# First value means written by ScalarE, keys sliced in three pieces, the projection one step sooner, waits per bank, spread weights in two buffers

## The chip, the cores and the metric

The kernel runs on one core of a Trainium2 chip. The metric is the device time of one execution in microseconds (us); less is better. The engines of the core are PE (TensorE, matmuls; PEld is its weight load), DVE (VectorE), ACT (ScalarE), POOL (GpSimd) and SP (SyncE, which here only issues DMAs). They run their own queues in order and meet at semaphores.

## The reference, cut to what matters

Three layers follow one another, on 2 batches of 768 rows:

```python
# 1: attention over a window of +-15 rows and 24 block summaries
k_sum = k.reshape(B, H, nb, block, D).max(axis=3)      # block = 32, nb = 24
v_sum = v.reshape(B, H, nb, block, D).mean(axis=3)
scores = concat(masked(scale * q @ k.T), scale * q @ k_sum.T + log(block))
x = softmax(scores) @ concat(v, v_sum)
# 2: four experts, each a causal attention with its own wq, wk, wv, wo; top 2 of 4 by a gate
for e in range(4):
    a = softmax(causal(scale * (x @ wq[e]) @ (x @ wk[e]).T))
    out += weight_of_expert(e) * (a @ (x @ wv[e]) @ wo[e])
# 3: token mixing, then channel mixing
u = out + (relu(out.T @ w_tok1) @ w_tok2).T
return u + relu(u @ w_ch1) @ w_ch2
```

## The kernel before, in words

**Order.** Batch 0 and batch 1 each run attention, projections, expert attention and token mixing (`sequence(b, more)`), then four groups of 384 rows run channel mixing (`group`). Each engine's program is written out by hand, step by step, with the step number k; what an engine does within a step, and so what waits behind what, is the order of the lines in its own `sequence`. Batch 0 is the one trip of a hardware loop (`Fori(0, B - 1)`), batch 1 is written out behind it.

**Attention, steps k = 2 to 15.** A unit u (0 to 11) is 128 query rows (t = u % 6) of four heads (q = u // 6, two pairs of heads). Here S(u), T(u) and V(u) are its scores (`a_scores`), its transposes (`a_transpose`) and its products with the values (`a_values`) on PE. At step k PE does S(k), T(k-2), V(k-3). DVE takes the maxima and normalises (`a_maxima`), ACT takes the exponentials (`a_exps`). ACT and DVE each copy half of the transposes (`a_to_sbuf`, tile PTA) and each write a half of the result in split precision: ACT XT_h (`a_x_hi`), DVE XT_l (`a_x_lo`), both for unit k-4. Semaphore `a_xl` counts the XT_l.

**Keys.** ACT copies windows of the keys KP, scaled, to KW (`key_windows`, L839, three pieces of four windows for each pair r, counted once by `a_kwin`). DVE adds block maxima (`key_maxima`). Pairs 2 and 3 are done at steps 3 and 4.

**Means of the values.** DVE sums blocks of VT (`value_sums`), PE turns the sums (`means`), ACT copies them scaled to VS, and SP sends VS by DMA to rows 96 to 119 of all 12 windows of VW (`place_means`, L329, waits for `a_vs`). For q = 0 this is done before step 2 (`a_first_means`, bank ps_o), for q = 1 at unit 5. V(0) and V(6) wait for the DMA (`ld_vs`). In SP's queue `load_keys(0, 3)`, the second half's queries and values and the weights stand behind `place_means(0, 0)`.

**Projections.** P0 to P7 (`m_project`) are 12 matmuls each: P0, P1, P4, P5 give queries, P2, P3, P6, P7 keys; P4 to P7 are for the second 384 rows and need XT of all 12 units (`a_xl`). Each result goes through ACT (`m_project_hi`, L870, two copies for queries, four for keys) and DVE (`m_project_lo`, L1072, as many). P0 is issued at step 13. Then come value products `m_value(0)` and `m_value(1)`.

**Expert attention, steps k = 0 to 16.** 14 units (`UNITS`), at step k scores(k), transposes(k-2), values(k-3). `m_weights` (DVE) writes the gate weight over the denominator, spread over 64 columns each, to the one buffer `wide`; `m_spread` (PE, then ACT) turns it to SPREAD; `m_normalise` (DVE) multiplies. All DVE work of `m_weights(0)` stands behind the gate's chain.

**Token mixing.** `m_token1`, `m_token2` on PE, `add_tokens` and `sum_x2` on DVE, `store_u` on ACT. The scores of units 0, 1 and 2 of the next batch are issued ahead of its tiles 2, 4 and 6, and behind the first of them `a_first_means(b + 1)`.

## Time and profile before

| | us |
|---|---|
| median of 3 runs | 492.0 (491.32 to 492.31) |
| profiled execution, its own time | 491.06 |
| its span, first to last instruction | 489.3 |
| PE busy | 450.5 (92%) |
| DVE busy | 249.3 (51%) |
| ACT busy | 191.1 (39%) |
| mean granted TensorE clock | 0.979 of full |

Busy times are sums over the whole span, which holds stages with different limits; the change touches those ahead of channel mixing.

### The profile page before, as it was taken

To read this page: it belongs to the slowest core of one execution; us is meant where nothing else is said; L and a number is where in the kernel's file an instruction comes from. 1 tells how busy PE (TensorE), PEld (TensorE's weight loads), DVE (VectorE), ACT (ScalarE), POOL (GpSimd) and SP (SyncE) were. 2 spreads that over 40 slices of the span, in tenths; PEclk is the share of its full clock that TensorE was granted. 3 is DMA by queue.
4 is the path that set the end of the run, shared out by engine and by line. 5 is a ranking of instruction groups with operands and counts; after the bars stand their busy time and mean duration, and the time that the engine had idled before them with its cause. 6 is when DMAs were issued, how large, how long until landed. Compare 5 with 4: busy or idle time off the path is not lost.

```text
span 489.3 us, 8326 instructions
## 1 busy us (share of the span) xinstructions
PE 450.5 (92%) x3254; PEld 382.8 (78%) x3254; DVE 249.3 (51%) x512; ACT 191.1 (39%) x574; POOL 29.1 (6%) x35
## 2 busy tenths in 40 slices
PE   7577989899978789898989999999999999999997
PEld 3355889587755569886868799889988999889985
DVE  4598483877647994848894565311212121212201
ACT  5468463655322885646771244201211021002200
POOL 3032960000000000000000000000000000000000
PEclk9599998999998999999999999999999999999999
DMA  8457371000383036000004550004001300020001
GB/s 281 127 178 176 109 256 68 1 2 0 98 269 110 3 89 261 1 0 1 2 1 129 201 188 1 8 36 150 2 0 44 118 32 0 21 76 32 0 23 43
DMA packets 19555, 38.38 MB, mean 78 GB/s; under 512 B 2112, under 2 KB 6592, under 8 KB 19520
## 3 DMA queue, kind: packets, MB, share of 16 engines
q1 hardware_dynamic: 17792, 34.75, 22.0%
q10 hardware_dynamic: 1728, 3.15, 1.7%
q8 instruction: 24, 0.39, 0.3%
q14 instruction: 11, 0.09, 0.1%
HBM read 30.42 MB, written 6.29 MB: 75 GB/s over the span
## 4 chain that ended last, share of the span: by engine, by line
PE 76%; DVE 14%; DMA 4%; issue 3%; ACT 2%; POOL 0%; ACTq 0%; DVEq 0%; POOLq 0%
PE ps_s L494 37%; PE ps_t L494 22%; PE ps_o L494 6%; PE ps_x L494 5%; DMA VW<-VS 3%; PE ps_t L632 3%; DVE KL L1072 2%; DVE nmaxA L1033 2%; DVE vsum L1180 1%; DVE PTA L1051 1%; DVE nmaxM L1122 1%; DVE ksum L1169 1%; DMA u_rows<-US 1%; ACT KH L870 1%; DVE US L1193 1%
## 5 line engine op out<-in xcount | busy, mean ns | idle before, releaser
L494 PE MATMUL ps_s<-UT_h,ch_h 128*128 128x384 f32 x192 | 65.0, 338 | 0.1
L494 PE MATMUL ps_s<-UT_h,ch_l 128*128 128x384 f32 x192 | 64.9, 338 | 0.0
L494 PE MATMUL ps_s<-UT_l,ch_h 128*128 128x384 f32 x192 | 64.9, 338 | 0.0
L1314 DVE SCALAR_TENSOR_TENSOR HID_l<-ps_s,HID_h 128x384 fp32r<-128x384 f32 x48 | 26.7, 557 | 66.0 <-ACT HID_h L1012 66.0
L1012 ACT ACTIVATE HID_h<-ps_s 128x384 fp32r<-128x384 f32 x48 | 23.6, 491 | 93.8 <-PE ps_s L494 93.7
L494 PE MATMUL ps_t<-ch_h,HID_h 128*128 128x512 f32 x144 | 56.7, 394 | 0.0
L494 PE MATMUL ps_t<-ch_h,HID_l 128*128 128x512 f32 x144 | 56.2, 390 | 0.0
L494 PE MATMUL ps_t<-ch_l,HID_h 128*128 128x512 f32 x144 | 56.1, 389 | 0.0
L1322 DVE TENSOR_TENSOR OS<-ps_t,UR 128x512 f32<-128x512 f32 x12 | 8.3, 691 | 83.6 <-PE ps_t L494 83.6
L829 ACT ACTIVATE PA<-ps_s,nmaxA 128x120 f32<-128x120 f32 x96 | 33.4, 375 | 19.4 <-DVE nmaxA L1033 19.4
L494 PEld LDWEIGHTS ps_s<-UT_h,ch_h 128*128 128x128 f32 x192 | 36.0, 188 | 0.6 <-DVE UT_l L1198 0.5
L494 PEld LDWEIGHTS ps_s<-UT_l,ch_h 128*128 128x128 f32 x192 | 36.1, 188 | 0.1
L885 ACT ACTIVATE PM<-ps_s,nmaxM 128x128 f32<-128x128 f32 (+5 forms) x48 | 30.1, 633 | 15.5 <-DVE nmaxM L1122 15.4
L494 PEld LDWEIGHTS ps_s<-UT_h,ch_l 128*128 128x128 f32 x192 | 36.0, 188 | 0.0
L1122 DVE TENSOR_REDUCE nmaxM<-ps_s 128x1 f32<-128x640 f32 (+5 forms) x28 | 26.7, 952 | 13.4 <-PE ps_s L494 13.4
L494 PEld LDWEIGHTS ps_t<-ch_h,HID_l 128*128 128x128 f32 x144 | 27.0, 188 | 5.8
L494 PEld LDWEIGHTS ps_t<-ch_l,HID_h 128*128 128x128 f32 x144 | 27.1, 188 | 5.3
L494 PEld LDWEIGHTS ps_t<-ch_h,HID_h 128*128 128x128 f32 x144 | 27.0, 188 | 5.3
L632 PE MATMUL ps_t<-ident,PM 128*128 128x128 f32 x168 | 23.3, 275 | 2.9 <-DVE PTM L1136 2.9
L547 PE MATMUL ps_t<-ident,PA 128*120 128x128 f32 x96 | 16.6, 300 | 9.2 <-DVE PTA L1051 3.8
L926 ACT ACTIVATE UT_h<-ps_o 128x512 fp32r<-128x512 f32 x8 | 4.8, 598 | 51.7 <-PE ps_o L711 47.8
L494 PE MATMUL ps_s<-KH,QS 128*128 128x512 f32 (+3 forms) x64 | 23.7, 376 | 0.0
(165 smaller groups left out, 909.7 us busy)
## 6 DMA issues: line engine op xcount, KB each, us to landing
VW<-in_vw SPq DMA_DIRECT2D x12, 384.0 KB, 8.2
KP<-in_kT SPq DMA_DIRECT2D x8, 384.0 KB, 6.8
QT<-in_qT SPq DMA_DIRECT2D x12, 256.0 KB, 5.3
VT<-in_vT SPq DMA_DIRECT2D x8, 384.0 KB, 6.8
u_rows<-US ACTq DMA_DIRECT2D x12, 256.0 KB, 2.1
ch_raw<-in_ch SPq DMA_DIRECT2D x4, 768.0 KB, 6.6
US<-u_rows SPq DMA_DIRECT2D x4, 768.0 KB, 5.8
ch_raw<-in_ch SPq DMA_DIRECT2D x12, 256.0 KB, 4.8
```

Source lines behind the costliest of these rows:

```text
L494: return pe.matmul(out, lhsT, rhs, start=start, stop=stop)
L547: last = pe.transpose(ps_t[0:KC, j // 2, (j % 2) * P:(j % 2 + 1) * P], PA[:, u % 3, j, :], ident[:, :])
L632: last = pe.transpose(ps_t[:, at_ // 512, at_ % 512:at_ % 512 + P], PM[:, u % 3, at_:at_ + P], ident[:, :])
L829: last = act.activation(PA[:, u % 3, j, :], ps_s[u % 2][:, j % 2, (j // 2) * KC:(j // 2 + 1) * KC], ACT.Exp, bias=nmaxA[:, u % 4, j:j + 1] ...
L870: last = act.activation((KH if key else QS)[own[(i + to) % 2], 2 * pair + i, n * GS:(n + 1) * GS], bank[g % 4][own[i], 0:GS], ACT.Copy, sc ...
L885: last = act.activation(PM[:, u % 3, part], ps_s[u % 2][:, :, :].rearrange("p a c -> p (a c)")[:, part], ACT.Exp, bias=nmaxM[:, t, e:e + 1 ...
L1012: act.activation(HID_h[:, m, :], bank[m % 4][:, 0:GS], ACT.Relu).then_inc(g_hh, 1)
L1033: dve.tensor_reduce(nmaxA[:, u % 4, :].rearrange("p (j r) -> p r j", r=2), ps_s[u % 2][:, :, 0:2 * KC].rearrange("p r (j c) -> p r j c", j=2),
L1072: last = dve.scalar_tensor_tensor(out, bank[g % 4][own[i], 0:GS], 1.0 if key else SCALE, hi, ALU.mult, ALU.subtract)
L1122: dve.tensor_reduce(nmaxM[:, t, experts[0]:experts[0] + n], ps_s[u % 2][:, :, :].rearrange("p a c -> p (a c)")[:, 0:n * stride] .rearrange ...
L1314: dve.scalar_tensor_tensor(HID_l[:, m, :], bank[m % 4][:, 0:GS], 0.0, HID_h[:, m, :].bitcast(F32), ALU.max, ALU.subtract).then_inc(g_hl, 1)
L1322: dve.tensor_tensor(OS[:, j, :], bank[4 + j % 2], UR[:, j, :], ALU.add).then_inc(g_o, 1)
```

## The change

What it does, by parts:

- **Start.** 16 warming matmuls in place of 20. The first query load holds 3 tiles of 128 rows, not 2. Values are loaded ahead of the rest of the queries. DVE sums the values of pair 0 and 1 between the maxima, in two parts.
- **First means.** `a_first_means` is issued at step 3, behind T(1), to bank ps_x. ACT writes the means itself to the first 4 windows (q = 0) or 2 windows (q = 1) of VW and then to VS; the DMA takes the other windows. V(0) and V(6) wait for ACT (`a_vd`), V(2t) from the first window on that the DMA writes waits for `ld_vs`; V(1) waits for `a_vs`.
- **Keys.** `key_windows` takes one piece of both pairs at a time, at steps 3, 4 and 5; scores wait for the piece that they read.
- **Projection.** P0 at step 12, P1 at 13, P2 at 14, P3 at 15. Waits for P0 and P2 are for their own bank and weights. Scores 0 and 1 of the experts wait for the bank that they overwrite, not for the last projection.
- **Spread weights.** `wide` has two buffers and lies in the weights' staging tile. The first spread and its normalisation are a step later, at 4.
- **Order at step 15.** The first `m_token1` goes ahead of transposes(13).
- **Loop.** Both batches are written out.

```diff
-N_WARM = 20
+N_WARM = 16
+CUT_AT = (3, 4, 5)
-Q_FIRST = 2 * P
+Q_FIRST = 3 * P
+DIRECT = (4, 2)
-SPREAD_AT = [LAST[_t] + 3 for _t in range(TQ)]
+SPREAD_AT = [LAST[_t] + (4 if _t == 0 else 3) for _t in range(TQ)]
...
+        wide = raw[:, :, 0:E * HD]
...
                 sp.wait_ge(a_vs, 2 * b + q + 1)
-                sp.dma_start(VW[WK:KC, q, :, :], VS[WK:KC, q, :].unsqueeze(1).broadcast_to([NB, NW, 4 * D])
-                             ).then_inc(ld_vs[q], 16)
+                sp.dma_start(VW[WK:KC, q, DIRECT[q]:NW, :],
+                             VS[WK:KC, q, :].unsqueeze(1).broadcast_to([NB, NW - DIRECT[q], 4 * D])).then_inc(ld_vs[q], 16)
...
             for r in range(2):
+                load_values(0, r)
+            for r in range(2):
                 load_queries(0, r)
-            for r in range(2):
-                load_values(0, r)
...
-            sp.wait_ge(a_kwin, B * PAIRS)
+            sp.wait_ge(a_kwin, B * PAIRS * 3)
...
-                    pe.wait_ge(a_kwin, b * PAIRS + 2 * q + 2)
                     pe.wait_ge(ld_qf[q], b * 16 + 16)
+                if t % 2 == 0:
+                    pe.wait_ge(a_kwin, b * PAIRS * 3 + 6 * q + t + 2)
...
-                means(ps_o, b, 0).then_inc(a_vm, 1)
+                means(ps_x, b, 0).then_inc(a_vm, 1)
...
                 if t == 0:
+                    pe.wait_ge(a_vd, 2 * b + q + 1)
+                if t == DIRECT[q] // 2:
                     pe.wait_ge(ld_vs[q], b * 16 + 16)
+                if u == 1:
                     pe.wait_ge(a_vs, 2 * b + 1)
...
+                if g % 2 == 0 and g < 4:
+                    pe.wait_ge(c_lo, g // 2 + 1)
+                    pe.wait_ge(a_exp, b * NU + NU - 1 + g // 2)
                 if g == 0:
                     pe.wait_ge(a_xl, b * NU + (NU - TQ // 2))
                 if g == 4:
...
-                if u == 0:
-                    pe.wait_ge(m_pl, b * 8 + 8)
+                if u < 2:
+                    pe.wait_ge(m_pl, b * 8 + 6 + 2 * u)
...
+                    if k == 3:
+                        a_first_means(b)
                     if 3 <= k <= NU + 2:
                         a_values(b, k - 3)
-                    if k == NU + 1:
-                        pe.wait_ge(c_lo, N_QK)
-                    if k > NU:
-                        m_project(b, k - NU - 1)
-
-                for g in range(3, 8):
+                    if k >= NU:
+                        m_project(b, k - NU)
+
+                for g in range(4, 8):
                     m_project(b, g)
...
+                    if k == SPREAD_AT[0]:
+                        m_spread(b, 0)
+                    if k == MU + 1:
+                        for m in range(KT):
+                            m_token1(b, 0, m)
                     if 2 <= k <= MU + 1:
                         m_transpose(b, k - 2)
                     if k - 1 in TURN_AT:
                         m_out_project(b, TURN_AT.index(k - 1))
-                    if k == MU + 1:
-                        for m in range(KT):
-                            m_token1(b, 0, m)
-                    if k in SPREAD_AT:
-                        m_spread(b, SPREAD_AT.index(k))
+                    if k in SPREAD_AT[1:]:
+                        m_spread(b, 1 + SPREAD_AT[1:].index(k))
...
                         a_scores(b + 1, SCORES_BEFORE.index(t))
-                        if t == SCORES_BEFORE[0]:
-                            a_first_means(b + 1)
...
-            with pe.Fori(0, B - 1) as b:
-                sequence(b, True)
-            sequence(B - 1, False)
+            for b in range(B):
+                sequence(b, b < B - 1)
...
+            def key_windows(b, q, i):
+
+                for r in (2 * q, 2 * q + 1):
+                    if i == 0:
+                        act.wait_ge(ld_k[r], b * 16 + 16)
+                    act.activation(KW[:, r, 4 * i:4 * i + 4, 0:WK], windows(r, 4 * i), ACT.Copy, scale=SCALE).then_inc(a_kwin, 1)
+
+            def a_means(b, q, sums):
+
+                n = DIRECT[q]
+                act.activation(VW[WK:KC, q, 0:n, :], sums.unsqueeze(1).broadcast_to([NB, n, 2 * P]), ACT.Copy,
+                               scale=1.0 / BLOCK).then_inc(a_vd, 1)
+                act.activation(VS[WK:KC, q, :], sums, ACT.Copy, scale=1.0 / BLOCK).then_inc(a_vs, 1)
...
                     if k <= NU + 1:
                         a_to_sbuf(b, k - 2)
+                    if k == 3:
+                        a_first_means(b)
                     if 3 <= k < NU:
                         a_exps(b, k)
-                    if k in KEYS_AT:
-                        key_windows(b, (2 + KEYS_AT.index(k),))
-                    if k > NU:
-                        m_project_hi(b, k - NU - 1)
+                    if k in CUT_AT:
+                        key_windows(b, 1, CUT_AT.index(k))
+                    if k >= NU:
+                        m_project_hi(b, k - NU)
...
-                if t >= 1:
-                    dve.wait_ge(m_d, b * TQ + t)
-                dve.tensor_tensor(wide[:, :].rearrange("p (e d) -> p e d", e=E),
+                if t == 0:
+                    dve.wait_ge(c_lo, N_TOK2)
+                if b * TQ + t >= 2:
+                    dve.wait_ge(m_d, b * TQ + t - 1)
+                dve.tensor_tensor(wide[:, t % 2, :].rearrange("p (e d) -> p e d", e=E),
...
-                    if k > NU:
-                        m_project_lo(b, k - NU - 1)
+                    if k >= NU:
+                        m_project_lo(b, k - NU)
...
+                    if k == SPREAD_AT[0]:
+                        m_normalise(b, 0)
...
-            a_maxima(0, 1, 0)
-            value_sums(0, (0, 1))
-            a_maxima(0, 2, 1)
+            a_maxima(0, 1)
+            value_sums(0, (0,))
+            a_maxima(0, None, 0)
+            a_maxima(0, 2)
+            value_sums(0, (1,))
+            a_maxima(0, None, 1)
```

## Rows read from the trace of the kernel before

**Rows 1.** Busy time in channel mixing: stretch, its length, PE, PEld, DVE, ACT, POOL, clock, DMA.

```profile
282.00:489.00 207.00, 203.95 (x1044) 186.09 (x1044) 51.75 (x87) 35.94 (x71) 0.00 (x0) 1.00 0.12 45
```

**Rows 2.** What PE waited for, 188 to 224 us: total, times, longest.

```profile
PE ps_x L647 <- DVE wide L1146: 1.7, 1, 1.7
PE ps_s L494 <- DVE KL L1072: 1.7, 1, 1.7
```

**Rows 3.** Busy times as in group 1: three stretches of equal length behind gaps of PE.

```profile
74.40:77.80 3.40, 3.40 (x18) 3.40 (x17) 0.69 (x1) 1.56 (x9) 0.00 (x0) 0.50 0.32 122
146.10:149.50 3.40, 3.40 (x9) 2.66 (x9) 1.29 (x2) 0.00 (x0) 0.00 (x0) 0.51 0.36 75
208.80:212.20 3.40, 3.40 (x31) 3.36 (x31) 0.69 (x1) 1.83 (x10) 0.00 (x0) 1.00 0.00 0
```

**Rows 4.** Timeline, attention of batch 0: start, us, instruction, idle before.

```profile
17.65 0.50 SPq L310 DMA_DIRECT2D KP<-in_kT  x1
21.83 1.15 PE L494 MATMUL ps_o<-PTA,VW 120*64 120x64 f32 x16 [3.07 <-DMA VW<-VS]
27.98 0.65 DVE L1033 TENSOR_REDUCE nmaxA<-ps_s 128x4 f32<-128x480 f32 x1
30.20 0.94 DVE L1180 TENSOR_REDUCE vsum<-VT 128x24 f32<-128x768 f32 x1
42.67 0.66 DVE L1033 TENSOR_REDUCE nmaxA<-ps_s 128x4 f32<-128x480 f32 x1 [0.94 <-PE ps_s L494]
```

**Rows 5.** DMA issues of 17.6 and of 21.5 us: KB, us to landing.

```profile
KP<-in_kT SPq DMA_DIRECT2D x1, 384.0 KB, 5.5
VT<-in_vT SPq DMA_DIRECT2D x2, 384.0 KB, 7.6
```

**Rows 6.** Groups of ACT by shape: count, busy us, mean ns, idle before.

```profile
L916 ACT ACTIVATE X_h<-ps_x 128x512 fp32r<-128x512 f32 x12 | 7.2, 596 | 9.8 <-PE ps_x L494 9.7
L850 ACT ACTIVATE VS<-ps_t 24x256 f32<-24x256 f32 x2 | 0.8, 377 | 3.5 <-PE ps_t L494 3.5
```

**Rows 7.** Timeline, token mixing of batch 0 and attention of batch 1.

```profile
145.04 0.62 PE L494 MATMUL ps_o<-ident,vsum 128*24 128x128 f32 x4 [2.50 <-DVE vsum L1180]
156.03 0.65 DVE L1033 TENSOR_REDUCE nmaxA<-ps_s 128x4 f32<-128x480 f32 x1
159.16 0.73 PE L494 MATMUL ps_o<-PTA,VW 120*64 120x64 f32 x16
178.13 0.66 DVE L1033 TENSOR_REDUCE nmaxA<-ps_s 128x4 f32<-128x480 f32 x1 [0.67 <-PE ps_s L494]
```

**Rows 8.** Timeline, batch 0: XT_l of unit 8, P0, P2, its copies, P4.

```profile
49.57 0.41 DVE L1058 TENSOR_TENSOR XT_l<-ps_o,XT_h 128x256 fp32r<-128x256 f32 x1
50.97 0.44 PE L494 MATMUL ps_s<-XT_h,wq_h 128*128 128x384 f32 x1
56.14 0.34 PE L494 MATMUL ps_s<-XT_h,wk_h 128*128 128x384 f32 x1
58.45 4.09 ACT L870 ACTIVATE KH<-ps_s 64x384 fp32r<-64x384 f32 x8 [0.72 <-PE ps_s L494]
60.47 4.56 DVE L1072 SCALAR_TENSOR_TENSOR KL<-ps_s,KH 64x384 fp32r<-64x384 f32 x8 [1.53 <-ACT KH L870]
60.36 0.34 PE L494 MATMUL ps_s<-XT_h,wq_h 128*128 128x384 f32 x1
```

**Rows 9.** Timeline, experts of batch 0: copy of transposes(1), then transposes(2).

```profile
90.44 0.68 DVE L1136 COPY PTM<-ps_t 128x512 f32<-128x512 f32 x1
91.22 0.85 PE L632 MATMUL ps_t<-ident,PM 128*128 128x128 f32 x6
```

**Rows 10.** Timeline, end of the experts of batch 0: transposes(13), their copy, the values.

```profile
125.82 0.87 PE L632 MATMUL ps_t<-ident,PM 128*128 128x128 f32 x6
126.73 0.69 DVE L1136 COPY PTM<-ps_t 128x512 f32<-128x512 f32 x1 [0.20 <-PE ps_t L632]
128.22 1.53 PE L494 MATMUL ps_o<-PTM,VE 128*64 128x128 f32 x24
```

More of the change, by code:

```diff
@@ L139, in program @@
         gate_rank = sb("gate_rank", [P, TQ, E], F32)
-        wide, end_wide = at("wide", [P, E * HD], F32, gate_at)
-        assert end_wide <= place[0]
         gate_w = sb("gate_w", [P, TQ, E], F32)
@@ L253, in program @@
         a_vsum = sem("a_vsum")
-        a_vm = sem("a_vm"); a_vs = sem("a_vs")
+        a_vm = sem("a_vm"); a_vs = sem("a_vs"); a_vd = sem("a_vd")
         a_s = sem("a_s")
@@ L646, in m_spread @@
                 for r in range(EP):
-                    last = pe.transpose(ps_x[:, r * P:(r + 1) * P], wide[:, r * P:(r + 1) * P], ident[:, :])
+                    last = pe.transpose(ps_x[:, r * P:(r + 1) * P], wide[:, t % 2, r * P:(r + 1) * P], ident[:, :])
                 last.then_inc(m_d, 1)
@@ L832, in a_exps @@
                 last.then_inc(a_exp, 1)
-            def key_windows(b, pairs):
-                for r in pairs:
-                    act.wait_ge(ld_k[r], b * 16 + 16)
-                    for w in range(0, NW, 4):
-                        last = act.activation(KW[:, r, w:w + 4, 0:WK], windows(r, w), ACT.Copy, scale=SCALE)
-                    last.then_inc(a_kwin, 1)
+            def key_windows(b, q, i):
[8 more added lines that the diff above has]
+                act.activation(VS[WK:KC, q, :], sums, ACT.Copy, scale=1.0 / BLOCK).then_inc(a_vs, 1)
             def a_first_means(b):
                 act.wait_ge(a_vm, b + 1)
-                act.activation(VS[WK:KC, 0, :], ps_o[WK:KC, 0:2 * P], ACT.Copy, scale=1.0 / BLOCK).then_inc(a_vs, 1)
+                a_means(b, 0, ps_x[WK:KC, 0:2 * P])
             def a_to_sbuf(b, u):
@@ L849, in a_to_sbuf @@
                 if u == MEANS_AT:
-                    act.activation(VS[WK:KC, 1, :], ps_t[WK:KC, 1, 2 * P:4 * P], ACT.Copy, scale=1.0 / BLOCK).then_inc(a_vs, 1)
+                    a_means(b, 1, ps_t[WK:KC, 1, 2 * P:4 * P])
                 if u >= 2:
@@ L978, in sequence @@
                 if more:
-                    key_windows(b + 1, (0, 1))
+                    for i in range(3):
+                        key_windows(b + 1, 0, i)
                 m_out_hi(b, TQ - 1)
@@ L998, in _ @@
             act.activation(sumA[:, 0, 0:1], denA[:, 0, 0:1], ACT.Exp)
-            key_windows(0, (0, 1))
+            for i in range(3):
+                key_windows(0, 0, i)
             for k in range(3):
                 a_exps(0, k)
-            a_first_means(0)
-            with act.Fori(0, B - 1) as b:
-                sequence(b, True)
-            sequence(B - 1, False)
+            for b in range(B):
+                sequence(b, b < B - 1)
             def group(g, more, first=False):
@@ L1223, in sequence @@
                         value_sums(b, (2 + SUMS_AT.index(k),))
-                    if k > NU:
-                        m_project_lo(b, k - NU - 1)
-                for g in range(3, 8):
+                    if k >= NU:
+                        m_project_lo(b, k - NU)
+                for g in range(4, 8):
                     m_project_lo(b, g)
@@ L1301, in _ @@
             a_maxima(0, 0)
-            a_maxima(0, 1, 0)
-            value_sums(0, (0, 1))
-            a_maxima(0, 2, 1)
-            with dve.Fori(0, B - 1) as b:
-                sequence(b, True)
-            sequence(B - 1, False)
+            a_maxima(0, 1)
[4 more added lines that the diff above has]
+            a_maxima(0, None, 1)
+            for b in range(B):
+                sequence(b, b < B - 1)
             def group(g, more, first=False):
```

20 lines of the change are left out of this document (9 added, 11 removed).

## The prediction

> **What bounds the kernel now.** I read the view by stage first. Channel mixing, from 282 us on, keeps PE busy 203.95 of 207 us at full clock [rows 1]; the change touches none of it. So the question is the 282 us ahead of it, and there the waits of PE and what ends them. In the timeline of attention (two stretches of some 30 us) DVE is the engine without a pause: maxima, normalising, copies and XT_l of one unit follow the last one's, and key maxima and value sums come on top. A gain of PE or ACT there counts only where DVE itself stood idle: 0.94 us behind V(6) in batch 0 and 0.67 in batch 1 [rows 4, 7], and at the start, where V(0) waited 3.07 us for the DMA of the means [rows 4]. In projections and experts PE sets the pace, with two waits in each batch, 1.7 us each: for the last KL ahead of the first scores, and for `wide` [rows 2]. In token mixing PE waited 2.50 us for value sums [rows 7].
>
> The sum is made against the profiled execution, 491.06 us (span 489.3). The median is 492.0.
>
> **The start and attention of batch 0: -1.2 us (from -4 to +1).** Fewer warming matmuls, values sooner and the new order of DVE bring V(0) ahead. Laid out with the durations of the trace, T(1) ends near 15.5 us, the means' matmuls near 16.4, ACT's direct write near 17.7, and V(0) starts there instead of at 21.83 [rows 4]: 4.1 us. But ACT's `a_vs` comes only then, near 18.0. SP's queue stands on it, and behind it `load_keys(0, 3)`, which was issued at 17.65 [rows 4] and landed 5.5 us later [rows 5]; now it is issued near 18.8 and lands near 24. At step 3 ACT now takes the first piece of both pairs, so it waits for that landing, with XT_h, PTA and all exponentials behind it. DVE comes to the maxima of unit 5 near 26.2 instead of 27.98 [rows 4], and next stands at the sums of VT, which are behind in the same SP queue: they were issued at about 21.6 and took 7.6 us [rows 5], and DVE used them at 30.20 [rows 4] with little to spare. The broadcast is a third smaller, which gives the queue back about what the later issue costs, so they land near 29.4. Left at unit 6: 0.7 us. At unit 5's means ACT writes two windows more, 512 elements a row: the row of that length takes 0.60 [rows 6], some 0.5 when instructions overlap. V(6) no longer waits, 0.94 of DVE's idle time [rows 4]. 0.7 - 0.5 + 0.94 makes 1.2. The upper end of the gain is V(0)'s whole 4.1, the lower a landing 2 us later than I put it.
>
> **Attention of batch 1: +1.4 (0 to +2.5).** Here the means were long ready; now they stand between T(1) and V(0). The matmuls take 0.6 [rows 7]. For ACT's write of 1,024 elements the trace has no row. From 256 elements in 0.38 to 512 in 0.60 [rows 6] it grows by 0.22 per 256, which gives 1.04; the bounds are 0.60 and twice that. So V(0) comes 1.7 us after its old place (159.16 less what came before) [rows 7], S(4) stands behind it, and DVE waits for S(4): 1.6 us less the little it had to spare. ACT's second direct write adds 0.45; the 0.67 of idle time behind V(6) goes [rows 7]. The keys in three pieces take the same 12 copies on ACT; the wait they save on PE lay beside a busy DVE, so nothing is counted.
>
> **Projections: +1.7 in each batch, +3.4 (-1.2 to +2.5 each).** P0 at step 12 needs XT_l of unit 8, which DVE ends at 49.98 [rows 8]; P0 began at 50.97. But T(11) and V(10) were already done then. P0, P1 and V(11) took 5.17 (50.97 to 56.14) and a product 2.11 (56.14 to 60.36 is two) [rows 8], so a V with its changes of shape is 0.95, and T is as long as the means' 0.6 [rows 7]. P0 at 50.05 + 2.11 + 0.6 + 0.95 + 2.11 + 0.95 puts P2 at 56.8, 0.6 us later than now. The large item is P4. It waits for XT_l of unit 11. That stands at step 15 of DVE's queue, and step 14 now holds the copies of P2, a key product: ACT starts its four copies 2.3 us after P2's first matmul (56.14 to 58.45) and takes 4.09/8 x 4 = 2.05, DVE then 4.56/8 x 4 = 2.28 and XT_l 0.41 [rows 8]. That is 7.1 us after P2's start; P3 ends 4.2 us after it (56.14 to 60.36) [rows 8]. PE stands 2.85 us ahead of P4, where it had no wait. Before, only the cheap copies of P1 stood there. Against this the first scores no longer wait for the last KL, 1.7 [rows 2]: they need the copies of P5, done two products sooner. 0.6 + 2.85 - 1.7 makes 1.7.
>
> **Spread weights: -0.1 each, -0.2 (0 to -1.5 each).** The wait of 1.7 for `wide` [rows 2] goes from its place, but DVE worked without pause through that stretch. Its copy of transposes(1) ends at 91.12, and transposes(2), which need it, began at 91.22 [rows 9]. PE now waits there.
>
> **Order at step 15: +0.65 each, +1.3 (0 to +1.4).** Before, `m_token1` (six matmuls, 1.4 us of the 2.40 between transposes(13) at 125.82 and the values at 128.22) covered their copy, 126.73 to 127.42 [rows 10]. Now the transposes begin 1.4 us later, their copy ends near 128.8, and the values at 128.9. The cover is gone, nothing is won.
>
> **Token mixing of batch 0: -4.3 (-2.7 to -4.8).** PE loses the wait of 2.50 and the 0.6 of matmuls [rows 7], and with them the low stretch that followed, 3.4 us at half the clock [rows 3], worth up to 1.7: 4.8 at most. DVE still does the sums there, so it sets what follows: added up through its queue, the maxima of unit 2 begin near 152.0 instead of 156.03 [rows 7]. The end of the loop, where PE waited for nothing that the trace shows, gives 0.3.
>
> **The clock: +2.0 (-1.4 to +2.0).** The granted clock has two levels here, 2.4 and 1.2 GHz. Behind the 1.7 us wait for KL it fell in batch 0 and not in batch 1 [rows 3]: in the same 3.4 us PE began 18 matmuls in the one and 31 in the other, so the fall cost 13/31 of 3.4, 1.4 us. It also fell behind the wait of 2.50. The stall ahead of P4, 2.85 us, is longer than both gaps, and what follows it is bound by PE. I take a fall in each batch, 3.4/2 = 1.7 of dense projections, less the 1.4 of before. The Trainium skill ("TensorE: Matmul & The Clock Gate", Part 1: The HAM clock gate) says that half the clock is the default and activity lifts it, and that a kernel with repeated idle gaps pays for the warming each time; by it the two new stalls cost this, and batch 1 of before was luck.
>
> **The sum.** -1.2 + 1.4 + 3.4 - 0.2 + 1.3 - 4.3 + 2.0 = +2.4 us, 493.5 us. The median stood 0.9 above the profiled execution; since the changed kernel is taken with both falls already, I add nothing for that.
>
> **Rivals.** *The clock holds in one batch or both.* The sum less 1.7 or 3.4: 491.8 or 490.1. For it: batch 1 held after 1.7 us [rows 3]. Against it: the longer gap. *The start keeps its gain* (the one on the faster side): ACT at step 3 finds pair 3's keys landed within about 3 us of their issue, and VT as early; then V(0)'s 4.1 reaches the units behind and the time is 493.5 - 2.9 = 490.6. It decides from a landing near 22 us. Against it stand the 5.5 and 7.6 us [rows 5]. *The new waits for DMA come last.* In batch 1 SP sends the windows from 4 on only after ACT's write, near 157. Batch 0's whole broadcast, issued just ahead of 17.65, held V(0) until 21.83 [rows 4]; at 4 to 5 us they land as V(2) wants them. With 1 us there and batch 0's VT a further 2 late, +3: 496.5. *The change does as it says and P4 is not held*: only if ACT and DVE drained P2's copies within P3, and 4.3 us of copies do not fit in 2.1; I give it no chance of its own.
>
> **Chances.** The forecast 0.42; clock kept in one batch 0.19, in both 0.11; start keeps its gain 0.15; DMA last 0.13. No change that this kernel's measurement can tell is within 0.2%, 1.0 us about 492.0. Faster takes the two cases at 490.1 and 490.6, slower the forecast but a small part and the last, same the case at 491.8 and that part. Range 489.9 to 496.0: from the case with the clock kept to just short of the DMA case. The forecast's own range is 492.4 to 495.0.
>
> **What would show it.** PE idle for 2 to 3 us ahead of P4 in both batches, ended by DVE's XT_l, with a low clock behind it; no wait for KL ahead of the first scores; PE waiting for DVE's PTM copy where it waited for `wide`; V(0) in batch 0 near 17.7 but exponentials of unit 4 only near 25, behind a wait of ACT for KP; V(0) of batch 1 behind ACT's write. It is wrong if P4 follows P3 without a gap, if ACT's write takes far from 1 us, or if KP and VT land sooner than now.

## The result, and the profile after

The changed kernel took 499.7 us (median of 4 runs, 497.37 to 501.9) against 491.7 (4 runs) of the kernel before on the same chip: ratio 1.0165, 95% interval 1.0107 to 1.0223. A second set of runs gave 499.35 us, ratio 1.015 (1.0127 to 1.0172). It is 8 us slower; I had forecast 2.4 in the sum and 1.5 against the median, in a range that ended at 496. The direction was right and the size was not.

The rows below are of the second profiled execution (499.63 us, span 497.8), which lies nearer to the median than the first (501.9 us). Channel mixing is what it was [rows 1]; stretch, length, PE, PEld, DVE, ACT, POOL, clock, DMA:

```profile
290.80:497.80 207.00, 203.80 (x1044) 185.94 (x1044) 51.51 (x86) 35.94 (x71) 0.00 (x0) 1.00 0.13 45
```

To see where the 8 us arise I took seven instructions of DVE that close a stage and set their starts side by side. The timeline of before (two more of them stand in [rows 8] and [rows 7]: XT_l of unit 8 at 49.57, maxima of unit 2 of batch 1 at 156.03):

```profile
80.65 1.22 DVE L1122 TENSOR_REDUCE nmaxM<-ps_s 128x4 f32<-128x1024 f32 x1 [4.92 <-PE ps_s L494]
132.69 0.68 DVE L1187 TENSOR_TENSOR US<-X_h,X_l 128x512 f32<-128x512 f32 x1
183.98 0.41 DVE L1058 TENSOR_TENSOR XT_l<-ps_o,XT_h 128x256 fp32r<-128x256 f32 x1
213.52 1.23 DVE L1122 TENSOR_REDUCE nmaxM<-ps_s 128x4 f32<-128x1024 f32 x1 [3.62 <-PE ps_s L494]
274.54 0.68 DVE L1198 TENSOR_TENSOR UT_l<-ps_o,UT_h 128x512 fp32r<-128x512 f32 x1
```

The same seven of the changed kernel:

```profile
46.99 0.41 DVE L1072 TENSOR_TENSOR XT_l<-ps_o,XT_h 128x256 fp32r<-128x256 f32 x1
79.60 1.22 DVE L1136 TENSOR_REDUCE nmaxM<-ps_s 128x4 f32<-128x1024 f32 x1 [3.08 <-PE ps_s L495]
134.44 0.68 DVE L1203 TENSOR_TENSOR US<-X_h,X_l 128x512 f32<-128x512 f32 x1
155.92 0.65 DVE L1047 TENSOR_REDUCE nmaxA<-ps_s 128x4 f32<-128x480 f32 x1
187.30 0.41 DVE L1072 TENSOR_TENSOR XT_l<-ps_o,XT_h 128x256 fp32r<-128x256 f32 x1
219.80 1.22 DVE L1136 TENSOR_REDUCE nmaxM<-ps_s 128x4 f32<-128x1024 f32 x1 [3.08 <-PE ps_s L495]
283.50 0.68 DVE L1214 TENSOR_TENSOR UT_l<-ps_o,UT_h 128x512 fp32r<-128x512 f32 x1
```

The differences of neighbouring starts, against the terms of my sum (the clock's +2.0 put where I had put it):

| stage, up to | before | after | change | forecast |
|---|---|---|---|---|
| start and attention 0, XT_l of unit 8 | 49.57 | 46.99 | -2.6 | -1.2 |
| projections 0, maxima of scores(1) | 31.08 | 32.61 | +1.5 | +2.0 |
| experts 0, first US | 52.04 | 54.84 | +2.8 | +0.55 |
| token mixing 0, maxima of unit 2 | 23.34 | 21.48 | -1.9 | -4.3 |
| attention 1, XT_l of unit 8 | 27.95 | 31.38 | +3.4 | +1.4 |
| projections 1, maxima of scores(1) | 29.54 | 32.50 | +3.0 | +3.4 |
| experts and token mixing 1 | 61.02 | 63.70 | +2.7 | +0.55 |
| sum | | | +9.0 | +2.4 |

**The wait ahead of P4 is there, the one for KL is gone.** What PE waited for from 193 to 231 us, the counterpart of [rows 2] (total, times, longest):

```profile
PE ps_s L495 <- DVE XT_l L1072: 2.7, 1, 2.7
PE ps_t L640 <- ACT PM L897: 1.8, 1, 1.8
PE ps_t L640 <- DVE PTM L1150: 0.4, 1, 0.4
```

**The clock fell in more places than I had counted.** Busy times as above: at P0 of batch 0, in attention of batch 1, in the experts of batch 0 and 1, and behind the wait ahead of P4 of batch 1:

```profile
47.60:51.00 3.40, 3.40 (x11) 3.40 (x12) 0.00 (x0) 0.00 (x0) 2.95 (x3) 0.52 0.42 151
156.00:166.20 10.20, 8.47 (x83) 5.80 (x84) 5.71 (x15) 6.70 (x27) 0.00 (x0) 0.53 0.17 47
92.00:95.40 3.40, 3.40 (x20) 2.22 (x17) 0.89 (x3) 1.46 (x5) 0.00 (x0) 0.52 0.00 0
231.20:234.60 3.40, 2.96 (x21) 2.10 (x18) 1.77 (x5) 2.92 (x8) 0.00 (x0) 0.59 0.00 0
201.42:204.82 3.40, 3.40 (x11) 3.40 (x12) 2.07 (x4) 0.00 (x0) 0.00 (x0) 0.55 0.00 0
62.60:66.00 3.40, 3.40 (x19) 3.40 (x20) 2.05 (x4) 0.97 (x2) 3.05 (x3) 1.00 1.01 282
```

The last row is P4 of batch 0: behind the same wait of 2.70 us the clock held there. In the first profiled execution of this kernel the same place was at half speed:

```profile
63.80:67.20 3.40, 3.35 (x10) 3.35 (x11) 2.12 (x4) 0.00 (x0) 2.14 (x2) 0.50 0.94 306
```

So the same program with the same wait pays for the fall in one execution and not in another, 10 matmuls started in 3.4 us against 19.

What a fall in the experts costs can be read too. In the run with the end of token mixing filled (below), whose experts have the same instructions, the clock held in both batches:

```profile
81.13:134.41 53.28, 48.62 (x400) 38.53 (x399) 38.17 (x81) 28.76 (x77) 0.00 (x0) 1.00 0.04 11
218.30:280.51 62.21, 57.25 (x441) 45.89 (x441) 46.14 (x93) 33.77 (x85) 0.00 (x0) 1.00 0.15 52
```

That is 53.28 us against 54.84 of the table in batch 0, and 62.21 against 63.70 in batch 1: 1.56 and 1.49 us.

**The start.** Timeline of batch 0, counterpart of [rows 4]:

```profile
15.88 1.02 ACT L850 ACTIVATE VW<-ps_x 24x1024 f32<-24x1024 f32 x1 [0.16 <-PE ps_x L495]
17.04 1.15 PE L495 MATMUL ps_o<-PTA,VW 120*64 120x64 f32 x16 [1.20 <-ACT VW L850]
18.24 1.40 SPq L311 DMA_DIRECT2D KP<-in_kT  x1
23.74 0.52 ACT L845 ACTIVATE KW<-KP 128x384 f32<-128x384 f32 x1 [4.66 <-DMA KP<-in_kT]
26.11 0.65 DVE L1047 TENSOR_REDUCE nmaxA<-ps_s 128x4 f32<-128x480 f32 x1
28.32 0.94 DVE L1196 TENSOR_REDUCE vsum<-VT 128x24 f32<-128x768 f32 x1
```

V(0) comes at 17.04, ACT waits 4.66 us for the keys and the maxima of unit 5 begin at 26.11; I had said 17.7, a wait, and 26.2. Only the values were sooner than I put them: the sum of VT began at 28.32 without a wait, 1.9 us ahead of its old place [rows 4], where I had left 0.7. The gain of the start differs between executions: the six traces with the same instructions up to there put XT_l of unit 8 from 45.72 to 48.36, which is 1.2 to 3.9 us ahead of before. And it does not need ACT's direct write: the run of start, key pieces and bank-wise wait (below), which places the means by DMA alone, has XT_l of unit 8 at 46.99 as well.

**Token mixing.** Timeline and, last, one DMA issue (KB, us to landing):

```profile
149.33 0.69 DVE L1203 TENSOR_TENSOR US<-X_h,X_l 128x512 f32<-128x512 f32 x1 [1.99 <-DMA u_rows<-US]
160.60 1.02 ACT L850 ACTIVATE VW<-ps_x 24x1024 f32<-24x1024 f32 x1 [0.60 <-PE ps_x L495]
161.76 1.14 PE L495 MATMUL ps_o<-PTA,VW 120*64 120x64 f32 x16 [1.20 <-ACT VW L850]
u_rows<-US ACTq DMA_DIRECT2D x1, 256.0 KB, 5.6
```

PE no longer waits for the value sums, but DVE now stands 1.99 us at its next sum, since that writes a buffer of US whose store landed only 5.6 us after its issue, while the loads of batch 1 shared the DMA engines. That takes back what PE gained. Most of the 1.9 us of the table is not the missing wait but the clock. The run with the projection part alone (below) keeps token mixing as it was before, with the same wait of 2.50, but there the clock held. Token mixing of before, and of that run:

```profile
132.69:156.03 23.34, 19.32 (x119) 14.04 (x118) 14.56 (x27) 5.12 (x20) 0.00 (x0) 0.93 0.70 216
142.44:164.23 21.79, 17.76 (x118) 12.87 (x118) 14.56 (x26) 5.13 (x20) 0.00 (x0) 1.00 0.82 232
```

So 1.55 of the 23.34 us were the low clock behind the wait, and against 21.79 the changed kernel's 21.48, also at full clock, is 0.3 us. Writing the loop out gave nothing: the run of the bank-wise wait alone, with the loop written out, took 23.37 there.

**Order at step 15.** The values of the last unit wait for the copy, as forecast (+0.7 us):

```profile
129.21 0.69 DVE L1150 COPY PTM<-ps_t 128x512 f32<-128x512 f32 x1 [1.64 <-PE ps_t L640]
129.96 1.53 PE L495 MATMUL ps_o<-PTM,VE 128*64 128x128 f32 x24 [0.56 <-DVE PTM L1150]
```

### The profile page after: what moved, and what is told of

Same layout as the page of the kernel before. It is cut to its first block, busy times and chain, and to the rows that moved or that the text cites. A ratio compares the mean times of both kernels' runs of the same rounds, so it can differ in the third digit from the quotient of the medians.

```text
span 500.1 us, 8325 instructions
## 1 busy us (share of the span) xinstructions
PE 457.7 (92%) x3250; PEld 388.4 (78%) x3250; DVE 250.5 (50%) x512; ACT 193.1 (39%) x578; POOL 28.5 (6%) x35
## 4 chain that ended last, share of the span: by engine, by line
PE 74%; DVE 15%; issue 5%; ACT 3%; DMA 2%; SPq 0%; ACTq 0%; POOL 0%; DVEq 0%; POOLq 0%
PE ps_s L495 36%; PE ps_t L495 21%; PE ps_o L495 7%; PE ps_x L495 6%; PE ps_t L640 2%; DVE nmaxA L1047 2%; DVE PTA L1065 1%; DVE nmaxM L1136 1%; DVE XT_l L1072 1%; DMA u_rows<-US 1%; DVE vsum L1196 1%; DMA KP<-in_kT 1%; DVE US L1209 1%; DVE KL L1086 1%; ACT KH L882 1%
## 5 line engine op out<-in xcount | busy, mean ns | idle before, releaser
L1136 DVE TENSOR_REDUCE nmaxM<-ps_s 128x1 f32<-128x640 f32 (+5 forms) x28 | 26.7, 953 | 10.6 <-PE ps_s L495 10.5
L495 PE MATMUL ps_o<-PTM,VE 128*64 128x128 f32 x336 | 24.5, 292 | 2.0 <-DVE PTM L1150 1.1
L549 PEld LDWEIGHTS ps_t<-ident,PA 128*120 128x120 f32 x96 | 11.3, 150 | 19.1 <-DVE PA L1057 10.9
```

The lines of the kernel that those rows point to most:

```text
L495: return pe.matmul(out, lhsT, rhs, start=start, stop=stop)
L549: last = pe.transpose(ps_t[0:KC, j // 2, (j % 2) * P:(j % 2 + 1) * P], PA[:, u % 3, j, :], ident[:, :])
L1136: dve.tensor_reduce(nmaxM[:, t, experts[0]:experts[0] + n], ps_s[u % 2][:, :, :].rearrange("p a c -> p (a c)")[:, 0:n * stride] .rearrange ...
```

## The experiments

Ratios are to the kernel before on the same chip, with 95% intervals. Where a stretch is given for batch 1, it is from the start of XT_l of unit 8 to that of the maxima of scores(1), as in the table: 29.54 before, 32.50 changed.

### Parts taken out of the changed kernel

**The changed kernel again.** No edit.

> The changed kernel as it is, to narrow its interval and to be the base of the three runs beside it. Both theories: ratio to before about 1.016 (499 to 500 us).

Measured: 499.35 us (497.88 to 500.04), 1.015 (1.0127 to 1.0172). It is the base of what follows.

**Without the projection part**, on PE, ACT and DVE alike, with P0 to P3 and their waits as before:

```diff
-                    if k >= NU:
-                        m_project(b, k - NU)
+                    if k > NU:
+                        m_project(b, k - NU - 1)
```

> The changed kernel with the projections back at their old steps (k > NU, no waits on the single splits). Theory A, the recorded sum: the part costs 1.7 us in each batch, so 3.4 us less than the changed kernel, and 2 to 3 us more if the low-clock stretches that follow P0 and P4 (46.7 to 53.5, 63.8 to 67.2 and 203.7 to 207.1 us in the trace of after) go too: 492 to 496 us. Theory B, the loss is in the spread step and the low clock that follows it: at most 1 us less than the changed kernel, 498 to 500 us.

Measured: 487.15 us, 0.9925 (0.9897 to 0.9953): 12.2 us less than the changed kernel, and faster than before. This part alone carries more than the whole loss; theory B fell, and the gain is larger than theory A had (492 to 496). Of it my sum held 0.6 and 2.85 in each batch and 2.0 for the clock, 8.9. By the traces (spans 497.8 and 485.1), 8.2 us less are in the projections of the two batches; most of the rest is in stretches that the edit does not touch, 1.6 in the experts of batch 0 and 1.4 in attention of batch 1, where the clock held, or was low for less time, in this trace. The stretch of batch 1 is 27.72:

```profile
179.88 0.41 DVE L1071 TENSOR_TENSOR XT_l<-ps_o,XT_h 128x256 fp32r<-128x256 f32 x1
207.60 1.22 DVE L1135 TENSOR_REDUCE nmaxM<-ps_s 128x4 f32<-128x1024 f32 x1 [3.08 <-PE ps_s L495]
```

**Without the spread part**: one buffer `wide` again, and

```diff
-SPREAD_AT = [LAST[_t] + (4 if _t == 0 else 3) for _t in range(TQ)]
+SPREAD_AT = [LAST[_t] + 3 for _t in range(TQ)]
...
-                    if k in SPREAD_AT[1:]:
-                        m_normalise(b, 1 + SPREAD_AT[1:].index(k))
+                    if k - 3 in LAST:
+                        m_normalise(b, LAST.index(k - 3))
```

> The changed kernel with the spread of query tile 0 back at step 3, the single buffer of the spread weights and the normalisation in its old place. Theory A, the recorded sum: the part gives 0.1 us in each batch, so the time stays within 0.5 us of the changed kernel. Theory B, from the trace of after, in which the stretch from the row maxima of scores(3) to out_project(0) grew by 1.9 us in batch 0 and 2.0 us in batch 1, with a wait of 1.83 us for the exponentials and a low clock from 94.5 to 97.9 us: about 4 us less than the changed kernel, 495 to 496 us.

Measured: 497.6 us (495.04 to 502.42), 1.012 (1.0075 to 1.0165). The interval overlaps that of the changed kernel: no more than a hint of 2 us, less than theory B wanted.

**Without the means part**: no direct writes, and

```diff
-                    if k == 3:
-                        a_first_means(b)
...
+                        if t == SCORES_BEFORE[0]:
+                            a_first_means(b + 1)
```

> The changed kernel with the first means back ahead of step 2 (before the loop, and in the token mixing of batch 0) and all means placed by DMA alone. Theory A, the recorded sum: the sum of values comes back into token mixing (4.3 us) and attention of batch 1 gets 1.4 us back: about 3 us more than the changed kernel. Theory B, from the trace of after: token mixing gained only 2.0 us and attention of batch 1 lost 2.5 us, so within 1 us of the changed kernel.

Measured: 499.55 us, 1.0167 (1.0136 to 1.0199). No difference, against my recorded 3 us. In its trace token mixing is back at 24.6 us and attention of batch 1 at 27.7: what the part gains in the one (3.2 us) it loses in the other (3.7). Much of both is the clock, which was low in this trace's token mixing from 146 to 153 us.

### The projection part by itself

**The projection part alone** on the kernel before (the loop over batches written out, as in the change).

> The kernel before with the projections one step sooner and their waits, and the batch loop written out; nothing else. Theory A (the part costs by itself: transposes and values of the last units fall between the projections, 0.6 us, and P4 waits 2.85 us for XT_l of unit 11, in each batch; the wait of 1.7 us for KL ahead of the first scores stays): about +7 us, and +1.5 us more for each stretch of low clock behind that wait: 499 to 502 us. Theory B (the cost comes only together with the earlier start and the other parts, as the trace without the part hints, since it is 12 us faster than the changed kernel): +3 us or less, at most 495 us.

Measured: 501.4 us (496.46 to 502.84), 1.0186 (1.0136 to 1.0237). Theory A. The part needs no help from the others. In batch 1 the stretch is 32.92, with the clock up throughout; PE there waited 2.71 us for XT_l ahead of P4, and 1.7 us for KL as before.

**XT of unit 11 ahead of the copies of projection 2**, in the changed kernel, on ACT and in the same way on DVE:

```diff
-                    if k >= NU:
+                    if k >= NU and k != NU + 2:
+                        if k == NU + 3:
+                            m_project_hi(b, 2)
                         m_project_hi(b, k - NU)
```

> The changed kernel, but ScalarE and VectorE make XT_h and XT_l of unit 11 ahead of their copies of projection 2. Theory A: XT_l of unit 11 is then ready 2 us before P4, the wait of 2.7 us in each batch is gone, and with it the low clock in P4 to P7 (1.5 us each): 8 us less than the changed kernel, 490.5 to 492 us. Theory C (the four copies of a key projection are themselves late, and P5 or P6 waits for a bank instead): 2 us less at most, 497 us.

Measured: 493.18 us (488.61 to 494.97, 11 runs), 1.0032 (1.0 to 1.0064): 6.2 us less than the changed kernel. The stall is the queue position of XT_l, as the prediction had it; the time lies between the theories, nearer to A. It is still 6 us above the kernel without the part. Most of that goes with the clock: three of the eleven executions took 488.6 to 489.9 us at a mean clock of 0.975 to 0.979, eight took 492.1 to 495.0 at 0.965 to 0.969.

**The wait ahead of P4 filled**: 12 matmuls on constants.

```diff
                 if g == 4:
+                    for _ in range(12):
+                        mm(ps_t[:, 0, :], ident_b[:, :], ident_b[:, :].unsqueeze(1).broadcast_to([P, 4, P]), True, True)
                     pe.wait_ge(a_xl, b * NU + NU)
```

> The changed kernel with 12 matmuls on constants (128x512 bf16, written to a bank that nobody reads) between P3 and the wait for XT_l of unit 11. Theory A, the low clock in P4 to P7 follows from the idle 2.7 us of TensorE: P4 and P5 take 4.4 us instead of 5.9 us in both batches and the time falls by about 3 us, to 496 us. Theory D, the falls come whatever TensorE does there: P4 and P5 take 5.9 us as before and the time is that of the changed kernel or up to 0.5 us more (499.4 to 500 us).

Measured: 497.56 us, 1.0137 (1.0102 to 1.0172), 1.8 us less. The interval overlaps that of the changed kernel, and theory A wanted 3 us with both batches at the low clock; so the cause is read from the trace. The stretch of batch 1 and the clock behind the fillers:

```profile
188.39 0.42 DVE L1075 TENSOR_TENSOR XT_l<-ps_o,XT_h 128x256 fp32r<-128x256 f32 x1
219.49 1.23 DVE L1139 TENSOR_REDUCE nmaxM<-ps_s 128x4 f32<-128x1024 f32 x1 [3.07 <-PE ps_s L496]
202.50:205.90 3.40, 3.40 (x19) 3.40 (x20) 2.07 (x4) 0.97 (x2) 0.00 (x0) 1.00 0.00 0
```

31.10 us: the wait is as long as it was, the clock is up, and 1.40 us are gone. So the price of this part in batch 1 comes apart. Without it 27.72; with XT_l in time (the run with both places mended, below) 28.13, so 0.41 for T(11) and V(10) among the projections; the stall 2.97; the clock 1.40.

**Without projection and spread parts.**

> The changed kernel without the projection part and without the spread part. Theory A, the recorded sum (spread -0.1 us in each batch): the same as without the projection part alone, 487.2 us. Theory B, from the traces: the stretch from the row maxima of scores(3) to those of scores(8) is 16.65 us without the spread part and 17.16 us with it where the clock stays up, 18.7 us where it falls: 0.5 to 2 us less in each batch, 483 to 486 us.

Measured: 488.67 us (486.23 to 493.08, 12 runs), 0.995 (0.9914 to 0.9986). No gain over 487.15, so not theory B; the intervals of the two runs overlap, and theory A's 487.2 is not excluded.

### What the other parts are worth

**The bank-wise wait alone** on the kernel before:

```diff
-                if u == 0:
-                    pe.wait_ge(m_pl, b * 8 + 8)
+                if u < 2:
+                    pe.wait_ge(m_pl, b * 8 + 6 + 2 * u)
```

> The kernel before with the first scores waiting bank by bank for the projections, and the batch loop written out; nothing else. Theory A, the recorded sum: the wait of 1.7 us for KL ahead of the first scores goes in each batch: 3.4 us less than before, 488 us. Theory E (the first scores start 1.7 us sooner, but the next ones wait for the last KL instead, and the clock falls as before): 1 us less at most, 490.5 us or more.

Measured: 489.87 us, 0.994 (0.9905 to 0.9976): 2.3 us less, between the theories. In the trace its 1.8 us are all there, 27.72 against 29.54:

```profile
183.16 0.41 DVE L1056 TENSOR_TENSOR XT_l<-ps_o,XT_h 128x256 fp32r<-128x256 f32 x1
210.88 1.22 DVE L1120 TENSOR_REDUCE nmaxM<-ps_s 128x4 f32<-128x1024 f32 x1 [3.08 <-PE ps_s L494]
```

**Start, key pieces and bank-wise wait**, the good half below. On the kernel before:

```diff
-N_WARM = 20
+N_WARM = 16
-Q_FIRST = 2 * P
+Q_FIRST = 3 * P
...
-                    if k in KEYS_AT:
-                        key_windows(b, (2 + KEYS_AT.index(k),))
+                    if k in CUT_AT:
+                        key_windows(b, 1, CUT_AT.index(k))
```

with the order of loads and of DVE's first maxima and sums as changed.

> The kernel before with the start (16 warming matmuls, three query tiles first, values ahead of the other queries, one sum of values between the maxima), the keys in three pieces, the bank-wise wait and the loop written out; without the projection, means, spread and order parts. Theory A, from the traces: 3.4 us by the bank-wise wait, 1 to 3 us by the start, and none of the 1.3 us of the order and of the 1 to 4 us of the spread: 484 to 486 us. Theory E: the start's gain is lost again behind the placing of the means by DMA, which is late as before: 488 us.

Measured: 485.74 us (484.8 to 487.88), 0.9875 (0.9828 to 0.9923). Theory A: these three are the good half of the change.

**Without projection part and order**: as the run without the projection part, and `m_token1(b, 0, m)` back in its old place at step 15.

```diff
-                    if k == MU + 1:
-                        for m in range(KT):
-                            m_token1(b, 0, m)
...
+                    if k == MU + 1:
+                        for m in range(KT):
+                            m_token1(b, 0, m)
                     if k in SPREAD_AT[1:]:
                         m_spread(b, 1 + SPREAD_AT[1:].index(k))
```

> The changed kernel without the projection part and with the first token product behind the spread again at step 15. Theory A, the recorded sum (order +0.65 us in each batch): 1.3 us less than without the projection part alone: 485.9 us. Theory F (the wait for the copy of the transposed scores only moves): 487.2 us, no difference.

Measured: 488.38 us, 0.9921 (0.9885 to 0.9956). Theory F's 487.2 lies in the interval, theory A's 485.9 does not. The 0.7 us of the order are in its trace (15.6 us from the maxima of scores(12) to the first US, 16.3 with the order), but not in the median.

**Without projection part and means.**

> The changed kernel without the projection part and with all means placed ahead of step 2 and by DMA alone. Theory A, the recorded sum (means -4.3 us in token mixing, +1.4 us in attention of batch 1): 3 us more than without the projection part alone, 490 us. Theory B, from the traces with and without the means part (token mixing 2.3 us shorter with it, attention of batch 1 2.3 us longer at the same clock, 3.7 us longer with the stretches of low clock): 0 to 1.5 us less, 485.6 to 487.2 us.

Measured: 488.73 us, 0.9931 (0.9898 to 0.9965). Between the theories, and not to be told from 487.15.

**The spread part on the good half.**

> The kernel of start, key pieces and bank-wise wait with the spread part. Theory A, the recorded sum: -0.1 us in each batch, 485.5 us. Theory B: 0.5 us more in each batch by the wait for the exponentials of scores(3) ahead of the transposes, and up to 1.5 us more in each by a fall of the clock behind it: 486.7 to 489.7 us.

Measured: 488.53 us (484.53 to 492.72, 12 runs), 0.9925 (0.989 to 0.996). Theory B in direction, though the intervals overlap (0.989 to 0.9923). In the traces batch 1's experts and token mixing take 61.51 us against 61.02, 0.5 more; batch 0's token mixing took 1.3 more, with a low clock from 139 to 149 us. This is where the 0.5 us come from. Timeline without the part (maxima of scores(3), normalisation of tile 0, values of tile 1):

```profile
216.68 0.95 DVE L1123 TENSOR_REDUCE nmaxM<-ps_s 128x2 f32<-128x768 f32 x1
218.89 0.41 DVE L1154 TENSOR_TENSOR OX<-ps_o,SPREAD 128x256 f32<-128x256 f32 x1
220.07 1.09 PE L495 MATMUL ps_o<-PTM,VE 128*64 128x128 f32 x16
```

With it:

```profile
217.57 0.95 DVE L1125 TENSOR_REDUCE nmaxM<-ps_s 128x2 f32<-128x768 f32 x1
219.19 0.68 DVE L1139 COPY PTM<-ps_t 128x512 f32<-128x512 f32 x1
219.97 0.84 PE L632 MATMUL ps_t<-ident,PM 128*128 128x128 f32 x6 [1.82 <-ACT PM L885]
220.92 0.41 DVE L1158 TENSOR_TENSOR OX<-ps_o,SPREAD 128x256 f32<-128x256 f32 x1
221.47 1.09 PE L493 MATMUL ps_o<-PTM,VE 128*64 128x128 f32 x16 [0.44 <-ACT PTM L897]
```

The transposes(2) begin 2.40 us behind the maxima with and without the part (219.08 without), at the end of DVE's copy of transposes(1), 219.87: so far the recorded sum, and the view's "ACT PM" is only the work that ended last by the profile. But the normalisation of tile 0 has moved from 2.21 us behind the maxima to 3.35, behind DVE's maxima of scores(4), and the values of tile 1 write the bank that it reads. They begin at 221.47, 3.90 us behind the maxima, instead of 3.39: 0.5 us. The view names ACT's copy of PTM there, which ended at 221.34, as the normalisation did at 221.33; but that is the copy of transposes(2), and by the program these values read transposes(1) and wait for the normalisation.

### The clock, and a better version

**The end of token mixing filled** in the changed kernel: 10 matmuls on constants ahead of the wait for the last sum.

```diff
                 if more:
+                    for _ in range(10):
+                        mm(ps_o[:, :], ident_b[:, :], ident_b[:, :].unsqueeze(1).broadcast_to([P, 4, P]), True, True)
                     pe.wait_ge(m_u, b * TQ + TQ)
```

> The changed kernel with 10 matmuls on constants ahead of the wait of 2.7 us for the last sum at the end of the token mixing of batch 0; nothing else. Theory A, the low clock of 156 to 167 us follows from this wait: it goes, and attention of batch 1 takes 28 us from the row maxima of unit 2 to XT_l of unit 8 instead of 31.4 us: 3 us less, 496 us. Theory D: it comes all the same, since the wait for the means and the short matmuls of attention are enough: 499 us.

Measured: 496.8 us, 1.0103 (1.0054 to 1.0152), 2.6 us less, with an interval that overlaps that of the changed kernel. It is theory A, though not its 28 us. The low stretch is gone, and attention of batch 1 takes 29.43 us instead of 31.38:

```profile
156.00:166.20 10.20, 7.60 (x122) 5.40 (x122) 7.70 (x18) 8.31 (x35) 0.00 (x0) 1.00 0.17 47
156.21 0.65 DVE L1049 TENSOR_REDUCE nmaxA<-ps_s 128x4 f32<-128x480 f32 x1
185.64 0.41 DVE L1074 TENSOR_TENSOR XT_l<-ps_o,XT_h 128x256 fp32r<-128x256 f32 x1
```

What stays, 29.43 less 27.95, is 1.5 us: my term of 1.4 for the means between T(1) and V(0).

**The good half with its long waits filled**: 6 and 8 such matmuls ahead of the value sums, 10 ahead of the placed means of batch 0, 5 at the end of token mixing. The first of the four places:

```diff
+                for _ in range(8 if b else 6):
+                    mm(ps_o[:, :], ident_b[:, :], ident_b[:, :].unsqueeze(1).broadcast_to([P, 4, P]), True, True)
                 pe.wait_ge(a_vsum, b * PAIRS + 2 * q + 2)
```

> The kernel of start, key pieces and bank-wise wait (485.7 us), with matmuls on constants (128x512 bf16, to a bank in no use) ahead of four waits: 6 and 8 ahead of the sums of values, 10 ahead of the placed means of batch 0, 5 at the end of the token mixing of batch 0. Theory A, the clock falls where TensorE has idled: the low stretches at 14 to 17, 20 to 24 and 143 to 146 us go, 3 us less: 483 us. Theory D, the falls come anyway, and the fillers reach past the waits: 0 to 1 us more, 486 to 487 us.

Measured: 483.87 us, 0.9819 (0.9772 to 0.9867), 1.9 us less than 485.74. The two intervals overlap, though the slowest of these six executions (484.33) is faster than the fastest of those (484.8).

**All waits of attention filled too**, 3 each for units 2 to 11:

```diff
+                    for _ in range(3):
+                        mm(ps_t[:, 0, :], ident_b[:, :], ident_b[:, :].unsqueeze(1).broadcast_to([P, 4, P]), True, True)
                 pe.wait_ge(a_norm, b * NU + (u + 1))
```

> As the run beside it, and 3 such matmuls ahead of the wait for the normalised scores of each of the units 2 to 11 in both batches. Theory A: the low stretch at 48 to 51 us goes too, 1.5 us less than the run beside it, if the fillers (0.64 us at full clock) hide in the waits of 0.7 to 1.5 us. Theory D: where the wait is shorter than 0.64 us the fillers delay the unit, up to 20 times 0.3 us: 3 to 6 us more than the run beside it.

Measured: 486.65 us, 0.9886 (0.9839 to 0.9932). Theory D: the clock is higher (0.993 against 0.989), but fillers that outlast their wait delay the work behind them: attention of batch 1 took 29.18 us, and 27.71 in the run before it, at full clock in both.

**Both places mended in the changed kernel** (XT of unit 11 first, end of token mixing filled).

> The changed kernel with XT_h and XT_l of unit 11 made ahead of the copies of projection 2, and with 10 matmuls on constants ahead of the wait at the end of the token mixing of batch 0. Theory A, the two mends add up (6.2 us and 2.6 us measured singly): 490.5 us, 1 to 2 us less than the kernel before. Theory G, the clock falls in another place once it is kept up here: 493 us, no gain over the first mend alone.

Measured: 488.85 us (487.7 to 492.9, 12 runs), 0.9948 (0.9912 to 0.9985). That is 10.5 us less than the changed kernel, and 0.5% faster than before. The two mends add up, as theory A had it; that they give more than 6.2 and 2.6 lies within the intervals. What the rest of the change costs, in the experts and in attention of batch 1, is less than its start and bank-wise wait give. In this trace the clock fell in attention of batch 1 all the same, some 4 us behind the filled wait (0.64 from 155.0 to 158.4), and attention took 30.50 us. The stretch of batch 1, 28.13:

```profile
181.69 0.42 DVE L1076 TENSOR_TENSOR XT_l<-ps_o,XT_h 128x256 fp32r<-128x256 f32 x1
209.82 1.22 DVE L1140 TENSOR_REDUCE nmaxM<-ps_s 128x4 f32<-128x1024 f32 x1 [3.08 <-PE ps_s L495]
```

**The good half, fillers ahead of `wide` as well** (7 in each batch, and 5 ahead of the waits for the normalised scores of units 9 to 11 of batch 0).

```diff
+                    for _ in range(7):
+                        mm(ps_x[:, :], ident_b[:, :], ident_b[:, :].unsqueeze(1).broadcast_to([P, 4, P]), True, True)
                 pe.wait_ge(m_den, b * (3 * TQ) + (3 * t + 3))
```

> The version with its long waits filled (483.9 us), and 7 such matmuls more ahead of the wait of 1.7 us for the wide weights in each batch and 5 ahead of the waits for the scores of units 9 to 11 of batch 0. Theory A: the low stretches at 44 to 51 and 85 to 88 us go, 482 us. Theory D: fillers (1.5 us and 1.1 us) that reach past their wait take it back: 484 us.

Measured: 482.12 us (480.94 to 482.59), 0.9786 (0.9743 to 0.983): the fastest of all, 2.1% under the kernel before, with an interval from 1.7 to 2.6%. Its page has no slice with a low clock (40 equal slices, tenths):

```profile
PEclk9999999999999999999999999999999999999999
```

## Why the prediction was right in direction and wrong in size

The direction was right by its mechanism: without the projection part the change is faster than before. The size was a miss of 6.6 us in the traces, +9.0 against +2.4.

- **The start, -1.2: measured -2.6** in this trace, and -1.2 to -3.9 over six. Each step up to unit 5 was right to 0.7 us. Mis-sized: the landing of VT, which I took to be at about 29.4; it was there by 28.3.
- **Projections, 0.6 + 2.85 - 1.7: measured in batch 1 +0.41 + 2.97 - 1.82.** The mechanism and its terms hold. What decided was the order of two copies in a queue, and moving them alone (6.2 us) shows it.
- **Spread weights, -0.1 each: measured +0.5.** I costed the buffer and left out the normalisation that moved with it. The values of tile 1 wait for it; this step of the part was not followed.
- **Order, +0.65 each: measured +0.7.** Right in the traces; too small for the medians.
- **Token mixing, -4.3: measured -1.9.** This step failed. Of the 1.9, 1.55 are the low clock that went, for which I had up to 1.7; of the other 2.6 us, 0.3 came. I followed DVE's queue with work alone and left out that its next sum waits for a store; the store had hidden behind the old wait. What was late next, once the stall was gone, was the store, 1.99 us. No run gives that sum another buffer, so that the store alone took the gain back is read from the trace, not shown by a run. The end of the loop, my 0.3, gave nothing.
- **Attention of batch 1, +1.4: measured +1.5 with the clock up.** ACT's write of 1,024 elements took 1.02 us; I had 1.04.
- **The clock, +2.0: this step failed most.** I counted one fall behind each new stall and took back those of before. Instead the clock fell in attention of batch 1 (2.0 us of time, shown by the run with the end of mixing filled), in the experts of both batches (1.56 and 1.49 us, by the trace in which it held there; the rest of their 2.8 and 2.7 is the 0.5 and 0.7 above), at P0 of batch 0 (1.5 us: the projections took 32.61, and 31.10 with the same terms and the clock up; PE had waited 1.88 us for XT_l there, but the good half, with P0 a step later, was low near that place too), and behind P4 in some executions only (1.40). That is some 7.9 us in the profiled execution, against 3.1 before (1.55 in token mixing, 1.5 in the projections of batch 0), 4.8 more. My sum held a net 0.3, the 2.0 less the 1.7 inside token mixing: this is 4.5 of the 6.6 us that it missed. Token mixing makes 2.3 more, the experts 1.3, and the start took 1.4 back. The Trainium skill ("TensorE: Matmul & The Clock Gate", Part 1: The HAM clock gate) says that half the clock is the default and that activity releases it. The filled waits agree: with no other change 485.7 us became 482.1. The same section puts the cost of the ramp at less than 1% of a typical kernel's span; here the falls come to more, 7.9 us in the changed kernel, 1.6% of 499.35.

None of my rivals held this case: each moved one mechanism, and the clock's falls came on top of all of them. What stays open is what decides whether it falls: behind the same wait of 2.70 us it fell in one execution and held in another, and behind the unchanged wait of 1.71 us for `wide` it fell in batch 0 of the good half, not in batch 1 and not in the kernel before. So part of what separates two profiled executions is which falls each happened to have.

## What to carry to other kernels

When a step is moved earlier, look at what its copies now stand in front of in the other engines' queues: here one XT_l behind a key product's copies cost 6 us over the two batches, and swapping the two gave it back. When a stall goes, look for waits that ended under its cover, stores into reused buffers above all. In the dense stages of this kernel, a wait of TensorE (they had 1.7 to 2.8 us here) is also a risk of 1.4 to 2.0 us of slow matmuls behind it, which varies from run to run; matmuls on constants that fit inside the wait took it away in most places, but three ahead of every wait of attention made the kernel slower (483.87 to 486.65 us). Before a stage's gain is put down to an edit, compare the clock of the two traces there.

## What the hardware showed that I had not expected

- Executions of one program can fall into groups by their mean clock. With XT of unit 11 first: 488.6 to 489.9 us at 0.975 to 0.979, 492.1 to 495.0 at 0.965 to 0.969. It is no strict order: the changed kernel took 499.07 us at 0.965 and 499.95 at 0.972.
- The low clock can last: 10.2 us at a mean of 0.53 in attention of batch 1 of the changed kernel, where PE was busy with short matmuls for 8.47 of them; with 2.33 us of matmuls on constants ahead of it the same 10.2 us ran at 1.00, on 7.60 us of PE's time.
- A store of 256 KB landed after 5.6 us while the loads of the next batch were under way.
